# Exchanging the real and imaginary half of a scan state by two DMAs instead of a matmul

## The reference

```python
# 1. complex linear recurrence, B,H,S,D = 2,8,768,48
scale = min(|a|, 0.999) / (|a| + 1e-6);  a = a * scale      # a = a_re + i a_im
for t in range(S):
    new_re = ar * S_re - ai * S_im
    new_im = ar * S_im + ai * S_re
    S_re, S_im = new_re + outer(k[t], v[t]), new_im
    y[t] = q[t] @ S_re
# 2. mixture of experts, 1536 tokens, 8 experts, capacity 384
e = argmax(x @ w_gate); gate = softmax(x @ w_gate)[e]
out = gate * (relu(x_e @ w1[e]) @ w2[e])                     # 384 -> 1024 -> 384
# 3. bilinear block: ((x @ w_a) * (x @ w_b)) @ w_out         # 384 -> 1536 -> 384
```

## Time and profile before

| | |
|---|---|
| time, median of 3 runs | 598.21 us (596.13 to 598.21) |
| profiled execution | 596.47 us, of which the span of the profile is 595.2 us |
| PE | busy 550.6 us, 93% of the span |
| DVE, ACT, POOL | busy 376.7, 269.1, 51.6 us |
| preparation | 0 to 120.8 us |
| chunk stage, units 0 to 31 | 120.8 to 218.8 us |
| first expert's rows turned and split | 218.8 to about 228 us |
| experts, bilinear block | to 595.2 us |

### The profile page before, as it was taken

How to read it: one execution, slowest core, us unless ns; L and a number is a source line. 1 busy time by engine, 2 the same in 40 slices (tenths; PEclk the granted TensorE clock), 3 DMA queues, 4 the chain that set the end, 5 groups by cost and what they waited for, 6 DMA issues and landing times.

```text
span 595.2 us, 10269 instructions
## 1 busy us (share of the span) xinstructions
PE 550.6 (93%) x3821; PEld 489.4 (82%) x3822; DVE 376.7 (63%) x937; ACT 269.1 (45%) x565; POOL 51.6 (9%) x66
## 2 busy tenths in 40 slices
PE   0499687889999999999999999999999999999996
PEld 0267355779999998999999998888888888888886
DVE  5999999978888878888888885444412212122121
ACT  5665657822222227777777784433331122322112
POOL 1000000001121116000000000350020000200002
PEclk9977899999999989999999999999999999999999
DMA  8998032497222124976666629720010000100001
GB/s 321 284 385 313 1 155 71 174 258 222 71 71 62 41 71 158 330 241 204 209 211 214 195 96 161 149 91 0 1 53 1 1 0 1 53 2 0 1 1 53
DMA packets 46322, 73.28 MB, mean 123 GB/s; under 512 B 16521, under 2 KB 38793, under 8 KB 45385
## 3 DMA queue, kind: packets, MB, share of 16 engines
q1 hardware_dynamic: 44360, 67.97, 37.3%
q0 software_dynamic: 1920, 4.75, 2.5%
HBM read 55.76 MB, written 16.97 MB: 122 GB/s over the span
## 4 chain that ended last, share of the span: by engine, by line
PE 82%; DVE 9%; ACT 5%; DMA 2%; issue 1%; POOL 0%; DVEq 0%; POOLq 0%; ACTq 0%; SPq 0%
PE psum L1311 25%; PE psum L1284 12%; PE psum L1117 11%; PE psum L1085 11%; PE psum L848 4%; PE psum L695 3%; PE psum L822 3%; PE psum L850 2%; PE psum L280 2%; PE psum L457 2%; PE psum L867 2%; PE psum L281 2%; DVE region L372 2%; DVE region L421 1%; PE psum L1038 1%
## 5 line engine op out<-in xcount | busy, mean ns | idle before, releaser
L1326 DVE TENSOR_TENSOR ga<-ga,psum 128x512 f32<-128x512 f32 x36 | 24.8, 688 | 129.8 <-PE psum L1311 129.8
L1330 ACT ACTIVATE gh<-ga 128x512 fp32r<-128x512 f32 x36 | 22.8, 632 | 82.0 <-DVE ga L1326 82.0
L1324 ACT ACTIVATE ga<-psum 128x512 f32<-128x512 f32 x36 | 21.5, 598 | 74.8 <-PE psum L1311 74.8
L1117 PE MATMUL psum<-hh,w2h 128*128 128x224 f32 x192 | 54.2, 282 | 0.0
L1085 PE MATMUL psum<-xh,w1h 128*128 128x224 f32 x192 | 53.1, 276 | 0.5 <-DVE xl L963 0.5
L280 PE MATMUL psum<-region,ident 128*128 128x384 f32 (+1 forms) x42 | 24.1, 663 | 31.0 <-ACT region L290 23.0
L1085 PE MATMUL psum<-xl,w1h 128*128 128x224 f32 x192 | 52.7, 274 | 0.0
L1085 PE MATMUL psum<-xh,w1l 128*128 128x224 f32 x192 | 52.7, 274 | 0.0
L1117 PE MATMUL psum<-hh,w2l 128*128 128x224 f32 x192 | 52.6, 274 | 0.0
L1117 PE MATMUL psum<-hl,w2h 128*128 128x224 f32 x192 | 52.6, 274 | 0.0
L1284 PE MATMUL psum<-woh,gh 128*128 128x384 f32 x144 | 48.3, 335 | 0.4 <-DVE gl L1332 0.4
(11 more groups left out here) (198 smaller groups left out, 1466.9 us busy)
## 6 DMA issues: line engine op xcount, KB each, us to landing
raw<-w SPq DMA_DIRECT2D x14, 1536.0 KB, 6.8
sorted_x<-region SPq DMA_DIRECT2D x8, 579.0 KB, 14.0
queries<-qk SPq DMA_DIRECT2D x4, 1152.0 KB, 25.5
xrow<-sorted_x SPq DMA_DIRECT2D x7, 579.0 KB, 4.0
region<-x_rows SPq DMA_DIRECT2D x14, 288.0 KB, 3.4
queries<-w SPq DMA_DIRECT2D x2, 1536.0 KB, 12.6
x_rows<-region SPq DMA_DIRECT2D x5, 576.0 KB, 2.8
region<-a SPq DMA_DIRECT2D x2, 1152.0 KB, 8.8
```

Of the source, the lines that this page charges most:

```text
L1117: m = nc.tensor.matmul(bank[YB0 + c][:, 0:cols], wx[:, f, c * P:(c + 1) * P], xx[:, f, 0:cols], start=f == 0 and i == 0, stop=f == NF - 1 ...
L1324: m = act.done(ss.activation(ga[f % 2][:], ba[:, 0:TT], ACT.Copy))
L1326: m = dve.done(tt(ga[f % 2][:], ga[f % 2][:], bb[:, 0:TT], ALU.mult))
L1330: m = act.done(ss.activation(gh[f % GB3][:], ga[f % 2][:], ACT.Copy))
```

## The change

It is made of these edits:

1. The matrix `swap` and its product are gone. After DVE's addition in `state_in(n)`, SP issues two DMAs from SBUF to SBUF (48 partitions x 224 fp32, 43 KB each), which write the imaginary rows where the real ones were and the other way round, into `zx[n % 2]`. SP first waits for the addition.
2. The product with Wr is now four ACT instructions (one for each head, 96x56, the factor as a scale per partition) that write a PSUM bank, 7 or 1 in turn.
3. `turned_state(n)` (wait for the two DMAs, multiply by Wi, add the product with Wr, write `Z`) now stands in the code of unit n+1, behind the addition of `state_in(n+1)`.
4. The sign that `swap` brought in is put into Wi: `ends` row 3 is written by two ACT instructions, one of them with scale -1 (for `ends` row 1 the operands are reordered), and the transposes L596 wait for them too.
5. V of the second batch is loaded in 4 parts, w1 in 6 and w2 in 8, one part per unit from unit 1 on.

```diff
+            zs = [flat(at, YB * DE, C2) for at in (AT_ZM, AT_ZM + YB * DE)]
+            zx = [flat(at, YB * DE, C2) for at in (AT_ZM + 2 * YB * DE, AT_ENDS)]
+            zr = [bank[i][0:C2, 0:YB * DE] for i in (7, 1)]
...
-            dve.done(vv.tensor_copy(ends[:, 2:4, :].rearrange("p i (r d) -> p i r d", r=2),
-                                    walk(AT_Z[1] + lo_at + D, [SA, 2], [0, 2], [1, D])))
+            dve.done(vv.tensor_copy(ends[:, 2, :].rearrange("p (r d) -> p r d", r=2),
+                                    walk(AT_Z[1] + lo_at + D, [0, 2], [1, D])))
+            act.wait(*m_step[HALF - 1])
+            act.done(ss.activation(ends[:, 3, 0:D], flat(AT_Z[2] + lo_at + D, D), ACT.Copy))
+            m_minus = act.done(ss.activation(ends[:, 3, D:C2], flat(AT_Z[2] + lo_at + D, D), ACT.Copy, scale=-1.0))
...
-            pe.wait(m_ends, *free[b])
+            pe.wait(m_ends, m_minus, *free[b])
...
                 m_add[n] = m
+                sp.wait_ge(dve.sem, m[1])
+                for i in range(2):
+                    sp.dma_start(zx[r][i * D:(i + 1) * D, :], zs[r][(1 - i) * D:(2 - i) * D, :]).then_inc(s_ex[r], 16)
+                n_ex[r] += 32
...
+            def turned_by_real(n):
+
+                act.wait(m_add[n], m_ends)
+                for i, p in enumerate(heads(n)):
+                    cut = slice(i * DE, (i + 1) * DE)
+                    m_zr[n] = act.done(ss.activation(zr[n % 2][:, cut], zs[n % 2][:, cut], ACT.Copy, scale=Wr[:, p:p + 1]))
+
             def turned_state(n):
-                pe.wait(m_add[n])
-                if m_turned_z:
-                    pe.wait(m_turned_z)
-                return pe.done(nc.tensor.matmul(bank[7][0:C2, 0:YB * DE], swap[:], zm[0], start=True, stop=True))
+                dve.wait(m_ends)
+                vv.wait_ge(s_ex[r], n_ex[r])
+                m = dve.done(tt(heads_of(zx[r]), heads_of(zx[r]), w, ALU.mult))
+                dve.wait(m, m_zr[n], m_y[n])
+                z_done[gr] = dve.done(tt(Z[gr], zr[r], zx[r], ALU.add))
...
+                if n in pieces:
+                    for y, x, s_ in pieces[n]:
+                        sp.dma_start(y, x).then_inc(s_, 16)
                 if more and n:
                     state_in(n)
+                if n > 1 and units[n - 1][0] < NC - 1:
+                    turned_state(n - 1)
...
                 if more:
-                    dve.wait(m_add[n], m_ends)
-                    m_zr = dve.done(tt(z3[1], z3[0], wv(Wr), ALU.mult))
+                    turned_by_real(n)
...
-                if more:
-                    m_j = turned_state(n)
-                    dve.wait(m_j)
-                    m_turned_z = m_jd[n] = dve.done(tt(z3[2], bank[7][0:C2, 0:YB * DE].rearrange("p (i e) -> p i e", i=YB),
-                                                       wv(Wi), ALU.mult))
-                    dve.wait(m_jd[n], m_zr, m_y[n])
-                    z_done[gr] = dve.done(tt(z3[3], z3[1], z3[2], ALU.add))
```

More of the change, by code:

```diff
@@ L122, in build @@
         baseb = sb("baseb", [L, E], BF16)
-        swap = sb("swap", [C2, C2])
+        sb("apart_left", [C2, C2])
         mask = sb("mask", [L, L])
@@ L138, in build @@
         m_ones = pool.done(g.memset(onesb[:], 1.0))
-        m = pool.done(g.memset(swap[:], 0.0))
-        pool.wait(m)
+        pool.wait(m_ones)
         c_id = pool.done(g.affine_select(out=ident[:], in_=ident[:], compare_op=ALU.not_equal, fill=1.0, base=0,
@@ L145, in build @@
                                           pattern=[[1, L]], channel_multiplier=-1))
-        c = pool.done(g.affine_select(out=swap[:], in_=swap[:], compare_op=ALU.not_equal, fill=1.0, base=-D,
-                                      pattern=[[-1, C2]], channel_multiplier=1))
-        pool.wait(c)
-        c_swap = pool.done(g.affine_select(out=swap[:], in_=swap[:], compare_op=ALU.not_equal, fill=-1.0, base=D,
-                                           pattern=[[-1, C2]], channel_multiplier=1))
         HALF = L // 2
@@ L621, in build @@
             maski = mask[:].bitcast(I32).unsqueeze(1).broadcast_to([L, YB, L])
-            zm = [flat(AT_ZM + i * YB * DE, YB * DE, C2) for i in range(3)]
+            zs = [flat(at, YB * DE, C2) for at in (AT_ZM, AT_ZM + YB * DE)]
+            zx = [flat(at, YB * DE, C2) for at in (AT_ZM + 2 * YB * DE, AT_ENDS)]
+            zr = [bank[i][0:C2, 0:YB * DE] for i in (7, 1)]
+            assert YB * DE <= 2 * P
             ws = [flat(AT_ENDS + i * P, P, C2) for i in range(2)]
@@ L646, in build @@
             pe.wait(*last)
+            act.wait(*(free[7] or ()))
             dve.wait(m_set, m_mask)
@@ L660, in build @@
             nc.tensor.wait_ge(s_vwin[0], 16)
-            pe.wait(c_swap)
             GB = NU // B
@@ L664, in build @@
             assert GB == XB and B == 2
-            m_scored, m_sc, m_u, m_y, m_yx, m_add, m_jd = ({} for _ in range(7))
+            m_scored, m_sc, m_u, m_y, m_yx, m_add, m_zr = ({} for _ in range(7))
+            s_ex = [sem(f"s_ex{i}") for i in range(2)]
+            n_ex = [0, 0]
             m_oh, m_slot, m_rk, m_tk, m_so, m_hot, m_part_x, m_read_lg = ({} for _ in range(8))
@@ L806, in build @@
                 load_x(i)
-            sp.dma_start(flat(AT_KQ, P // 2 * D, L), v[1]).then_inc(s_v[1], 16)
             sp.wait_ge(s_vw[1], 16)
-            sp.dma_start(flat(AT_VW[1], VWN, L), vw_rows[1]).then_inc(s_vwin[1], 16)
+            s_w0 = sem("s_w0")
+            y1, y2 = raw_0[0].rearrange("p (c f) -> p c f", c=KC), raw_0[1].rearrange("p (f n) -> p f n", f=NF)
+            x1, x2_ = w1[0].rearrange("(c p) f -> p c f", p=P), w2[0].rearrange("(f p) n -> p f n", p=P)
+            VP = 4
+            VCUT = P // 2 * D // VP
+            parts = [(flat(AT_KQ + i * VCUT, VCUT, L), v[1][:, i * VCUT:(i + 1) * VCUT], s_v[1]) for i in range(VP)]
+            parts.append((flat(AT_VW[1], VWN, L), vw_rows[1], s_vwin[1]))
+            WP = 2 * KC
+            cuts = [(c, slice(h * F // 2, (h + 1) * F // 2)) for c in range(KC) for h in range(2)]
+            parts += [(y1[:, c, cut], x1[:, c, cut], s_w1 if i == WP - 1 else s_w0) for i, (c, cut) in enumerate(cuts)]
+            parts += [(y2[:, f, :], x2_[:, f, :], s_w2 if f == NF - 1 else s_w0) for f in range(NF)]
+            pieces = {n + 1: [x] for n, x in enumerate(parts)}
+            assert len(parts) < NUNIT - 2 * GB
             scores(0)
@@ L896, in build @@
                     m_ends = end_factors()
-                z3 = [x.rearrange("p (i e) -> p i e", i=YB) for x in (*zm, Z[gr])]
-                def wv(x):
-                    return x[:, gr * YB * NC + j:(gr + 1) * YB * NC:NC].unsqueeze(2).broadcast_to([C2, YB, DE])
                 if more:
-                    dve.wait(m_add[n], m_ends)
-                    m_zr = dve.done(tt(z3[1], z3[0], wv(Wr), ALU.mult))
+                    turned_by_real(n)
+                if n == 1:
+                    turned_state(0)
                 if n:
```

23 lines of the change are left out of this document (14 added, 9 removed).

## The result

| | before | changed |
|---|---|---|
| time in one comparison | 597.43 us (596.13 to 598.21, 4 runs) | 610.04 us (606.78 to 631.57, 4 runs) |
| ratio | | 1.0194 (1.0160 to 1.0229) |
| span of the profiled execution | 595.2 us | 608.8 us |
| mean granted clock of the profiled execution | 0.979 | 0.958 |

The ratio leaves out the run of 631.57 us; why the runs differ so much is the subject of what follows. Predicted were 590.5 us, faster; the kernel is slower by 1.9% (1.6 to 2.3%), and one of its four runs by 5.7%.

What follows compares the result with a forecast made beforehand. PE was taken as the bound, DVE next. From the profiled 596.5 us, -11.1 (swap), +1.0 (preparation) and +3.7 (end) gave 590.1; predicted 590.5, own range 588 to 592.5, 8 in 10 from 587 to 598.5.

Steps and rivals of the forecast that it cites:

- The swap leaves PE: Chunk stage: 23 swaps of 0.41 us, 9.4, plus 2.1 at the first units, less 0.4: gain 11.1 us.
- The DMA wait on DVE: Even units of the chunk stage: the exchange wait is covered by PE's 5.50 us loop up to L = 1.81; cost zero.
- L = 1.6: Landing time in us of an exchange's second DMA, taken near the store's; lower bound 1.3.
- the loop 3.69 + L: DVE's loop once in two units, from addition through exchange landing to choose: 3.69 us plus landing time L.
- rival A: Chunk stage: small DMA lands in 2.1 us, DVE bounds a pair at 5.79, 3.5 us lost, 593.6; chance 0.27.
- The odd unit: Exchange queued behind load_x lands some 3.2 us after the addition began, covered by 3.48 us of DVE work: nothing paid.
- The start gain of 2.1 us: Units 0 to 2: three swaps and two PE waits for DVE, 2.3 us, go; 2.1 taken.
- The clock: End of stage only: last queried may run at 1.2 GHz, 1.36 us more, of which 0.5 was taken.
- The preparation: Before the chunk stage: two ACT copies come first and delay the factor copy-out, +1.0 us (0.8 to 1.2).
- The end: End of stage: unit 29's exchange lands behind the rows' load, delaying the last queried: +3.7 us (3.2 to 4.6).
- C: Rival, end of stage: unit 29's exchange not held behind the rows' data, term 1.6 us smaller or more, 588; chance 0.13.

Runs made afterwards that it cites:

- e11: Changed kernel with DVE doing masked and place_chunk before the state products, and unit 29's exchange issued before the rows' load: 592.66, 594.93, 630.86 and 631.97 us.
- e1: Changed kernel with V of the second batch and expert 0's weights loaded in one piece each, exchange kept: 637.34 us, ratio 1.0666.
- e17: Changed kernel with three orders altered (early ACT end copies, unit 29's exchange before the rows' load, masked and place_chunk before state products), no dummy product: 624.57 us.
- e20: As e17, plus a dummy PE product, its result never read, in units 0 to 4: 600.39 us.
- e12: Changed kernel without the two exchange DMAs and the wait for them, so the exchange is left out of the computation: 587.53 us, ratio 0.9815.
- e6: Changed kernel with a dummy PE product, result never read, as many columns as the swap, in the swap's place: 602.59 us, ratio 1.0108.
- e9: Changed kernel with DVE doing masked(n+1) and place_chunk before the state products: 600.9 us, ratio 1.0065.
- e19: As e12, but the exchanges of units 0 to 3 are issued and waited for: 594.35 us (594.14 to 598.73).
- e3: Changed kernel with SP loading the first expert's rows behind the exchange of unit 29 instead of ahead: 620.55 us (608.27 to 631.89).
- e14: Changed kernel with load_x and the weight parts issued by ScalarE on its own DMA queue: 630.5 us (612.06 to 653.4).
- e10: As e17, plus load_x issued behind its unit's exchange: 626.42 us (594.71 to 629.82).

## Why the prediction was wrong, by its steps

The prediction's terms came to -6.4 us of span; measured were +13.6. The 20 us between them are, from the table: 6.1 of waits for the exchange in the stage, put at nothing (2.0 up to unit 4, 3.1 up to unit 14, 1.0 from unit 19 to 30); 7.4 of the clock between units 14 and 19, put at nothing; 2.2 more at the end of the stage; 2.7 after it, put at nothing; 1.0 at its start; 0.5 of the swap. So two steps failed: the wait for the exchange, which was to be covered by other work of DVE, and the unspoken one that PE, as the bound, keeps its full clock through the stage.

**The swap leaves PE: right.** Predicted -11.1 us in the stage; with the exchange taken out it is -10.6 us (the four rows from unit 0 to 30, second column of the table), and in the profile of `e11`, exchanges in place and clock up, -7.4.

**The DMA wait on DVE: mis-sized, and this step failed.** It had "issues two DMAs (0.32 us each as the store was the earlier trace rows)" and L = 1.6, so 1.98 us from the first issue to the product. Measured: 0.59 us an issue and 1.9 us of landing, 2.5 us in a unit with nothing else on the queue:

```profile
216.11 1.14 SPq L853 DMA_DIRECT2D region<-region  x2
...
218.59 0.39 DVE L898 TENSOR_TENSOR region<-region 96x224 f32<-96x224 f32 x1 [0.28 <-DMA region<-region]
```

By the loop 3.69 + L that acts as L = 2.1, rival A: pair 5.8. In units 19 to 30, where little else is on the queue, the changed kernel loses 1.0 us to the one without exchange in 11 units: 0.2 us a pair, so A was right about the even units. The Trainium skill, "DMA: Bandwidth & Descriptors", "Anatomy of one DMA", gives about 2.0 us fixed for DMAs that GpSimd issues. The median of 1.9 is near it, for a DMA of 42 KB from SBUF to SBUF that SP issues, which is not the kind it names.

**The odd unit: wrong.** "Nothing is paid", since 3.2 us were covered by 3.48. Behind a weight part and `load_x` it took 5.1 us from the issue to the product (160.01 to 165.12). The part had been called "through before the next", on a store's pace alone; in most windows of the first batch the DMA engines are at 0.6 to 0.85 share, not the 0.26 of the earlier trace rows. Between units 4 and 14 it is 3.1 us against no exchange.

**The first units: missed.** The start gain of 2.1 us came (-2.2 from unit 0 to 2) and went again by unit 4 (+2.3), while the exchange of unit 0 takes 3.7 us from issue to product (126.62 to 130.30) and the first loads run. Without exchanges only 0.3 of it went again, so 2.0 are theirs.

**The clock: the step that I did not have.** The prediction took the clock for a term of 0.5 us at the end. It fell in the middle, behind waits of 1 to 2 us; all waits of the first batch by themselves cost 5 us, and the clock cost 7.4 us between units 14 and 19 in the profiled run (+6.7 against -0.7), some 28 to 30 where it fell by unit 3 (`e1`, 28.6 from unit 3 to 17; `e17` against `e20`, 29.5). That is why no case of mine reached 610 or 631: each priced a wait at its length. That exchange waits bring the fall is shown (`e12`, and the dummies of `e6`, `e20`). What decides in a given run is not: `e9` fell in no run, `e11` in half of its runs and `e17` in all, with first waits of 1.24, 1.40 and 1.56 us, which looks like an order by size, but the first wait of `e19` was 1.94 and it fell in none, and the profiled changed kernel had 1.99 and fell 37 us later.

**The preparation: nearly right.** Predicted +1.0. L597 comes at 110.61, 1.59 us behind the start of L403, against 0.43 for L600 before: +1.2. This distance is 1.58 or 1.59 in every profile with the copies in this place, and 0.43 with the copies early. The whole stage start was 2.0 late; the rest is not the change's: L403 itself came at 109.02, against 108.06 for its like before (L410), ahead of the edit.

**The end: mechanism right, too small.** Predicted 6.7 us from R (SP's issue of the rows' load) to `turn_first`, the exchange held behind that load; measured 229.74 - 221.51 = 8.2. L898 waited 4.83 us, its exchange was usable 3.8 us behind its first issue, and `queried(31)` then ran at 0.50 (2.6 us instead of 1.36). R came 1.5 us late instead of 0.3. Together +5.9 instead of +3.7; C is refuted. `e3` and `e11` show that swapping two issues on SP ends it (+1.7 in this stretch in both).

## What to carry to other kernels

When a change takes filler work off the bounding engine and puts a latency in its place, price the latency twice: by its length, and by what happens to the clock if that engine then stands for a microsecond or two. Where the granted clock sits at 0.50 and the engine is fully busy, look for the first idle time ahead of that stretch, not for more work in it. And write an exchange's latency as two issues plus a landing measured on its own kind, behind everything that the same queue and the same DMA engines carry in that very unit.

## What was not expected of the hardware

- PE kept at 1.2 GHz while busy without a gap, for 54 us and more (`e17`: 132 to 186 us, 54.00 of 54.00 busy by the profile's account, clock 0.50), and came back at about units 17 to 19, behind the last chunk of the first batch, in each profile whose clock fell in that batch. In `e14` it fell again in the second batch and stayed at 0.50 there (218 to 250 us, busy all the time). The Trainium skill, "TensorE: Matmul & The Clock Gate", section "HAM oscillation — how this bites in real kernels", describes waits for DMAs after which the clock drops. These traces show such drops too, behind shorter waits than its example has (1.27 to 2.22 us in nine of the ten falls). That a busy PE gets its clock back, which the same page has in "Part 1: The HAM clock gate", does not hold in the stretch of `e17` above, as far as the profile's busy time tells.
- The same binary gave 592.66 and 631.97 us (`e11`), and 594.71 and 629.82 (`e10`), on one core and one chip.
- An exchange DMA of 42 KB within SBUF took SP 0.50 us at the least and 0.59 in the median to issue, against 0.32 for a store of 576 KB and 0.43 for `load_x`.
